# Splitting the columns of each batch 512 + 256 instead of 384 + 384 in a linear-attention, expert and feed-forward kernel

## The chip, the cores and the metric

One NeuronCore of a Trainium2 chip runs the program. The metric is device microseconds for one execution; the median of three runs is given beside the profiled execution. Engines are called PE (matrix products), DVE (vector), ACT (scalar), POOL (GpSimd) and SP (the queue that issues most transfers).

## The reference

```
# q, k, v: 2 batches, 8 heads, 768 places, 64 wide; blocks of 64 places
intra = (q_b @ k_b^T) * lam**(i - j)            # inside a block, i >= j
out_b = intra @ v_b + (q_b * lam**(i+1)) @ state
state = lam**64 * state + (k_b * lam**(63-i))^T @ v_b
x = out, heads side by side                     # 1536 tokens x 512
p = domain_probs / (sum + 1e-9)                 # 4 experts
x = sum_e p_e * (relu(x @ w1[e]) @ w2[e])       # 512 -> 1024 -> 512
h = x @ w_in;  out = (h * cos(h)) @ w_out       # 512 -> 2048 -> 512
```

All of it is in 32-bit floats. The kernel handles attention in 6 blocks of 128 places (`BLOCKS`), each for 2 batches (a unit is one block of one batch, 12 in all).

## The kernel before

Every number that goes into a product of the two later stages is split into a high part, rounded to the fast 32-bit matmul format, and a low part that is what is left. A product is then three matmuls: high by high, low by high, high by low. Copies to the high part are made by ACT, subtractions for the low part by DVE or POOL. All engines wait on semaphores by hand-written counts; the order on each engine is the order of the code.

**Attention.** DVE first makes two decay tables by running products along 128 places (`tensor_tensor_scan`): eight scans for `dmask`, from which `kpow` is copied, and four for `qpow`. Their input `lam` is loaded by ACT's queue while SP's queue loads q, k and v. Then, by block pairs p = 0 to 5, PE runs `scores`, `from_state`, `from_scores`, `decayed_state` and `increment`; DVE multiplies scores by the mask (`mask`, line 624) and makes parts of x and of the sums of x (`x_parts`, lines 645 to 653); ACT makes high parts (`x_high`, `t_high`); POOL multiplies q by `qpow` (`q_decay`, line 339) and makes low parts of the sums (`t_low`, line 345). The weights of the first quarter are split into high and low between these (`w1_piece`, lines 438 and 659).

**Experts.** The hidden width of the four experts is walked in 16 quarters of 256. The first product of a quarter is a seven-product form of a 2 by 2 block product (P1, P6, P5, P2, P7, P4, P3, in this order), on x and on sums of its blocks; the sums are why the columns (tokens) come in two batches. Before, the 768 columns of a batch were two sides of 384, and a step is one side of one quarter: 32 steps. A step holds 7 first products of 6 matmuls each (line 962) and, between them, the second products (`down`, line 981) of the step before, 8 of 6 matmuls each, 384 columns wide. Which of these follow which first product is written out in `FOLLOW` (and `FOLLOW_LAST` for the last step). Three PSUM banks hold the seven products, five are a ring for the second products. ACT copies P1 from its bank to memory (line 517), DVE adds it to P6 and P7 (lines 730 and 757), makes the four results (lines 715), applies relu and the expert's share (line 720), and adds second products to `y` (`down`, line 700). ACT makes the results' high parts (line 504), POOL their low parts (`h_low`, line 406). PE waits at the head of a product: P6 of side 1 for both pieces of the second weights (`w2_count(q, 1)`), P7 for DVE's sum with P6, P4 for DVE's sum with P7, and so on.

**Feed-forward.** 48 products of 4 x 3 matmuls of 512 columns (line 1040), each with two second products of 512 columns (line 1059). Their input is `y` of the experts, split again (`x2_high`, `x2_low`). The first of them waits for all low parts of the first side, of which DVE makes the second batch (line 706) and POOL the first. The eight second products of the last expert step stand among the first two of the 48.

```
FOLLOW = ((), (), (0,), (1, 2), (3, 4), (5, 6), (7,))
FOLLOW_LAST = ((), (0, 1), (2, 3), (4, 5), (6, 7), (), ())
```

## Time and profile before

| | |
|---|---|
| median of 3 runs | 826.63 us (826.59 to 828.08) |
| profiled execution | 826.41 us, its span 824.6 us |
| PE busy | 810.4 us (98% of the span), 4788 matmuls |
| DVE busy | 586.1 us (71%) |
| ACT / POOL busy | 291.5 us / 235.6 us |
| attention | 0 to 51.7 us |
| experts | 51.7 to 549.4 us |
| feed-forward | 551.4 us to the end |

A matmul is shown with an end that is modelled, and the next one starts before it, so that the time one costs is the distance between starts and not the duration shown. The list of stages above is read off the starts of lines 962 and 1040.

### The profile page before, as it was taken

Reading aid. Unit: us, or ns where it says so; the run is one execution under the profiler, and the core shown is the slowest. Engines: PE = TensorE matmul, PEld = TensorE weight load, DVE = VectorE, ACT = ScalarE, POOL = GpSimd, SP = SyncE. Lnnn points to the kernel's source line nnn. Section 1 sums busy time; section 2 is a strip of 40 time slices with the busy share of each in tenths; the row PEclk is TensorE's granted clock in tenths of the full one; section 3 lists DMA queues with packets and bytes.
Section 4 is the critical chain, followed back from the end, with each engine's and each line's share of the span. In section 5 each row is a group of like instructions: output and inputs, shape, how many; then the busy total and the mean of one; then the engine's idle time right before and its main releaser. Section 6 shows DMA issues by size and latency. Waiting matters only on the chain.

```text
span 824.6 us, 12232 instructions
## 1 busy us (share of the span) xinstructions
PE 810.4 (98%) x4788; PEld 757.7 (92%) x4788; DVE 586.1 (71%) x1028; ACT 291.5 (35%) x552; POOL 235.6 (29%) x232
## 2 busy tenths in 40 slices
PE   8988999999999999999999999999999999999998
PEld 7878999999999999999999999988888888888886
DVE  5987767667667667667667667676777777877776
ACT  3742322222222222221221222246545455454542
POOL 3854443443442442442442442243000000000000
PEclk9999999999999999999999999999999999999999
DMA  8941211111111021011011011100001101110004
GB/s 302 325 144 52 65 27 39 36 68 40 29 36 39 26 77 39 26 39 39 27 38 40 27 28 40 36 27 22 30 27 39 39 26 34 30 39 27 1 0 153
DMA packets 19869, 44.88 MB, mean 54 GB/s; under 512 B 2344, under 2 KB 2392, under 8 KB 19812
## 3 DMA queue, kind: packets, MB, share of 16 engines
q1 hardware_dynamic: 19668, 44.10, 17.0%
q8 instruction: 38, 0.62, 0.3%
q14 instruction: 19, 0.16, 0.1%
q10 hardware_dynamic: 144, 0.01, 0.0%
HBM read 40.93 MB, written 3.17 MB: 53 GB/s over the span
## 4 chain that ended last, share of the span: by engine, by line
PE 93%; DVE 4%; issue 1%; DMA 1%; ACT 0%; DVEq 0%; SPq 0%
PE ps L981 32%; PE ps L962 28%; PE ps L1040 16%; PE ps L1059 16%; DVE att L624 1%; DMA att<-att_in 1%; PE ps L879 1%; DMA lam<-lam_in 1%; PE ps L929 0%; DVE att L609 0%; DVE x_lo L706 0%; DVE w_lo L664 0%; DVE temps L715 0%; DVE temps L720 0%; PE ps L916 0%
## 5 line engine op out<-in xcount | busy, mean ns | idle before, releaser
L406 POOL TENSOR_TENSOR h_lo<-temps,h_hi 128x384 fp32r<-128x384 f32 x128 | 137.4, 1074 | 298.7 <-ACT h_hi L504 295.9
L504 ACT ACTIVATE h_hi<-temps 128x384 fp32r<-128x384 f32 x128 | 67.3, 526 | 360.1 <-DVE temps L720 360.1
L700 DVE TENSOR_TENSOR y<-ps,y 128x384 f32<-128x384 f32 x240 | 132.4, 554 | 72.5 <-PE ps L981 71.8
L981 PE MATMUL ps<-h_hi,w_hi 128*128 128x384 f32 x512 | 171.2, 334 | 0.0
L981 PE MATMUL ps<-h_hi,w_lo 128*128 128x384 f32 x512 | 171.1, 334 | 0.0
L981 PE MATMUL ps<-h_lo,w_hi 128*128 128x384 f32 x512 | 171.1, 334 | 0.0
L962 PE MATMUL ps<-x_hi,w_hi 128*128 128x384 f32 x448 | 150.9, 337 | 4.3 <-DVE w_lo L664 2.5
L962 PE MATMUL ps<-x_lo,w_hi 128*128 128x384 f32 x448 | 150.3, 335 | 0.0
L962 PE MATMUL ps<-x_hi,w_lo 128*128 128x384 f32 x448 | 150.3, 335 | 0.0
L981 PEld LDWEIGHTS ps<-h_lo,w_hi 128*128 128x128 f32 x512 | 96.1, 188 | 0.1
L981 PEld LDWEIGHTS ps<-h_hi,w_hi 128*128 128x128 f32 x512 | 96.1, 188 | 0.1
L981 PEld LDWEIGHTS ps<-h_hi,w_lo 128*128 128x128 f32 x512 | 96.1, 188 | 0.0
L962 PEld LDWEIGHTS ps<-x_hi,w_hi 128*128 128x128 f32 x448 | 84.6, 189 | 5.8 <-issue 3.0
L962 PEld LDWEIGHTS ps<-x_lo,w_hi 128*128 128x128 f32 x448 | 84.5, 189 | 0.0
L962 PEld LDWEIGHTS ps<-x_hi,w_lo 128*128 128x128 f32 x448 | 84.5, 189 | 0.0
L839 DVE SCALAR_TENSOR_TENSOR temps<-temps,ps 128x512 f32<-128x512 int32 x48 | 33.0, 687 | 61.5 <-ACT temps L582 61.5
L1040 PE MATMUL ps<-x_hi,w_hi 128*128 128x512 f32 x192 | 74.8, 389 | 1.7 <-DVE x_lo L706 1.7
L1059 PE MATMUL ps<-h_hi,w_hi 128*128 128x512 f32 x192 | 74.8, 390 | 0.0
L1040 PE MATMUL ps<-x_hi,w_lo 128*128 128x512 f32 x192 | 74.8, 390 | 0.0
L1040 PE MATMUL ps<-x_lo,w_hi 128*128 128x512 f32 x192 | 74.8, 389 | 0.0
L1059 PE MATMUL ps<-h_lo,w_hi 128*128 128x512 f32 x192 | 74.8, 389 | 0.0
L1059 PE MATMUL ps<-h_hi,w_lo 128*128 128x512 f32 x192 | 74.7, 389 | 0.0
(83 smaller groups left out, 1120.6 us busy)
## 6 DMA issues: line engine op xcount, KB each, us to landing
w_raw<-w_in SPq DMA_DIRECT2D x96, 256.0 KB, 2.6
att<-att_in SPq DMA_DIRECT2D x24, 512.0 KB, 6.3
temps<-p_scr SPq DMA_DIRECT2D x4, 768.0 KB, 4.1
out<-y SPq DMA_DIRECT2D x12, 256.0 KB, 2.0
att<-dp_in SPq DMA_DIRECT2D x1, 24.0 KB
p_scr<-att SPq DMA_DIRECT2D x1, 24.0 KB
lam<-lam_in ACTq DMA_DIRECT2D x1, 6.0 KB, 4.7
```

The lines of the kernel that those rows point to most:

```text
L406: pool.tensor_tensor(hs_lo[:, s % 2, f, at], r_ring[:, n % R_RING, :], f32(hs_hi[:, s % 2, f, at]), ALU.subtract).then_inc(s_hlo, 1)
L504: act.activation(hs_hi[:, s % 2, f, CT * b:CT * (b + 1)], r_ring[:, n % R_RING, :], ACT.Copy).then_inc(s_hhi, 1)
L624: dve.tensor_tensor(masked[:, n % 2, par, :], ps[:, (2 * n + par) % S_BANKS, :], dmask[:, par, :, :].rearrange("p a n -> p (a n)"), ALU.mu ...
L700: dve.tensor_tensor(at, from_bank, at, ALU.add).then_inc(s_y, 1)
L839: dve.scalar_tensor_tensor(out=rr[:, t, :], in0=kf[:, t, :], scalar=-C1, in1=bank, op0=ALU.mult, op1=ALU.add).then_inc(s_r1, 1)
L879: mm = pe.matmul(ps[:, (2 * n + par) % S_BANKS, at], qk[own, s, 1, at], qk[own, s, 0, at], start=True, stop=True)
L962: mm = pe.matmul(ps[:, bank, 0:CT], ww[q % 2][:, of], xx[:, side, 2 * x + k, :], start=(opens and k == 0 and n == 0), stop=(k == 1 and n = ...
L981: mm = pe.matmul(ps[:, DOWN_BANK + g % DOWN_BANKS, 0:CT], ww[:, s // SIDES % 2, f, at], hh[:, s % 2, f, tokens], start=(f == 0 and n == 0) ...
L1040: mm = pe.matmul(ps[:, v % GATE_BANKS, :], ww[q % 2][:, of], xx[:, k, chunk(c)], start=(k == 0 and n == 0), stop=(k == KT - 1 and n == 2))
L1059: mm = pe.matmul(ps[:, GATE_BANKS + i % KT, :], ww[:, q % 2, f, at], hh[:, j % CHUNKS, f, :], start=(f == 0 and n == 0), stop=(f == 1 and ...
```

## The change

The sides become 512 and 256 columns of each batch: blocks 0 to 3 are side 0, blocks 4 and 5 side 1. A first product has 512 columns on side 0 and 256 on side 1. The second products of a step are taken over both batches together in pieces of 512 columns: 8 for side 0 (two pieces of columns by four of outputs), 4 for side 1. So a quarter has 84 first matmuls as before, half of 512 and half of 256 columns, and 72 second ones of 512 in place of 96 of 384. In the feed-forward nothing changes but where its input's high and low parts are made: each chunk of 512 columns is now awaited by itself.

Other edits: the load of `lam` is the first on SP's queue; the four `qpow` scans come after `mask(0)`, `mask(1)` and `k_decay(1)`; POOL runs `normalise` and two `q_decay` before `diag`; on DVE the last piece of the first weights, `w1_piece(0, 2)`, comes after `mask(11)`; on ACT `t_high(4)` comes after the copy of P1 of step 0; in step 0 the pieces of the second weights are split earlier; on side 1 PE waits for the second weights at P5, not P6; `FOLLOW_LAST` is gone.

```
-CT = SEQ // SIDES
+SIDE_BLOCKS = (4, 2)
+CTS = (512, 256)
+CT = 512
...
-FOLLOW = ((), (), (0,), (1, 2), (3, 4), (5, 6), (7,))
-FOLLOW_LAST = ((), (0, 1), (2, 3), (4, 5), (6, 7), (), ())
-DOWN = KT * BATCH
+FOLLOW = (((), (), (), (0,), (1,), (2,), (3,)), ((), (), (0,), (1,), (2, 3), (4, 5), (6, 7)))
+DOWNS = (8, 4)
...
+            sp.dma_start(lam[:, :], lam_in).then_inc(s_lam, 16)
             load_qk(0)
...
+            normalise()
+            pool.wait_ge(s_tab, PAIRS)
+            q_decay(2)
+            q_decay(3)
             pool.wait_ge(s_id, 1)
...
-            act.dma_start(lam[:, :], lam_in).then_inc(s_lam, 16)
...
-                if p:
+                if 0 < p < BLOCKS - 1:
                     t_high(p - 1)
-                if 0 < p < BLOCKS - 1:
                     new_state(p)
...
                 if s == 0:
+                    t_high(BLOCKS - 2)
                     t_high(BLOCKS - 1)
+                    w2_piece(0, 0)
                     h_high(s, 0)
-                    w2_piece(0, 0)
+                    w2_piece(0, 1)
                     h_high(s, 1)
...
+            for a in range(PAIRS):
+                dve.tensor_tensor_scan(qpow[:, a, :], lam[:, HEADS + a:HEADS + a + 1].to_broadcast([P, P]),
+                                       zeros, 1.0, ALU.mult, ALU.add).then_inc(s_tab, 1)
             mask(2)
...
-                if 2 <= p <= 4:
+                if 2 <= p <= 3:
                     w1_piece(0, p - 2)
                 if p + 1 < BLOCKS:
                     mask(2 * p + 3)
+                if p == 4:
+                    w1_piece(0, 2)
...
-                    mm = pe.matmul(ps[:, bank, 0:CT], ww[q % 2][:, of], xx[:, side, 2 * x + k, :],
+                    mm = pe.matmul(ps[:, bank, 0:CTS[side]], ww[q % 2][:, of], xx[side][:, 2 * x + k, :],
...
-                    pe.wait_ge(s_hlo, 4 * s + 3 + b)
+                    pe.wait_ge(s_hlo, 4 * s + (3 if side == 0 and b == 0 else 4))
...
-                    mm = pe.matmul(ps[:, DOWN_BANK + g % DOWN_BANKS, 0:CT], ww[:, s // SIDES % 2, f, at],
-                                   hh[:, s % 2, f, tokens], start=(f == 0 and n == 0), stop=(f == 1 and n == 2))
+                    mm = pe.matmul(ps[:, DOWN_BANK + g % DOWN_BANKS, :], ww[:, s // SIDES % 2, f, at],
+                                   hh[side][:, f, tokens], start=(f == 0 and n == 0), stop=(f == 1 and n == 2))
...
-                            pe.wait_ge(s_xlo, UNITS // SIDES * (side + 1))
-                            pe.wait_ge(s_tlo, BLOCKS // SIDES * (side + 1))
+                            pe.wait_ge(s_xlo, 2 * sum(SIDE_BLOCKS[:side + 1]))
+                            pe.wait_ge(s_tlo, sum(SIDE_BLOCKS[:side + 1]))
...
-                    if i == P6 and side == 1:
+                    if i == P5 and side == 1:
 
                         pe.wait_ge(s_wlo, w2_count(q, 1))
...
-                        pe.wait_ge(s_x2lo, KT * (c + 1))
+                        if c != 1:
+                            pe.wait_ge(s_x2lo, KT * (c // 2 + 1))
+                        else:
+                            pe.wait_ge(s_x2lo1, KT)
                     if v == 0:
-                        pe.wait_ge(s_x2lo1, KT)
                         pe.wait_ge(s_r, 4 * STEPS - 3)
```

Three places on DVE, in the order of its queue. The first is its start: before, the scans for `dmask` (L609), the copy to `kpow` (L612), the scans for `qpow` (L616), and then the masks (L624) and `k_decay` (L633). The scans are listed as SCALAR_TENSOR_TENSOR.

```order
L609 SCALAR_TENSOR_TENSOR att<-lam,att 128x128 x8
L612 COPY kpow<-att 128x8
L616 SCALAR_TENSOR_TENSOR att<-lam,att 128x128 x4
L624 TENSOR_TENSOR att<-ps,att 128x512 x4
L633 TENSOR_TENSOR att<-att,kpow 128x512
```

The same stretch of the changed kernel (its lines: L623 and L626 are the `dmask` scans and the copy, L633 the masks, L642 `k_decay`, L679 the `qpow` scans):

```order
L623 SCALAR_TENSOR_TENSOR att<-lam,att 128x128 x8
L626 COPY kpow<-att 128x8
L633 TENSOR_TENSOR att<-ps,att 128x512 x4
L642 TENSOR_TENSOR att<-att,kpow 128x512
L679 SCALAR_TENSOR_TENSOR att<-lam,att 128x128 x4
```

The `qpow` scans moved behind the first two masks and `k_decay(1)`. The second place is the end of the attention on DVE, before: `mask(10)`, the last piece of the first weights (L659), `mask(11)`, then `x_parts(4)`.

```order
L653 TENSOR_TENSOR x_lo<-ps,x_hi 128x2x128
L624 TENSOR_TENSOR att<-ps,att 128x512 x2
L659 TENSOR_TENSOR w_lo<-w_sum,w_hi 128x1024
L624 TENSOR_TENSOR att<-ps,att 128x512 x2
L645 TENSOR_TENSOR att<-att,ps 128x256
```

And changed, where L668 is that piece:

```order
L662 TENSOR_TENSOR x_lo<-ps,x_hi 128x2x128
L633 TENSOR_TENSOR att<-ps,att 128x512 x4
L668 TENSOR_TENSOR w_lo<-w_sum,w_hi 128x1024
L654 TENSOR_TENSOR att<-att,ps 128x256
L655 TENSOR_TENSOR att<-ps,att 128x256
```

The piece now stands behind both masks. The third place is step 0 and the start of step 1 on DVE. Before: the sum with P6 (L730), result 0 (L720), the sum with P7 (L757), result by result (L715, L720), and the two pieces of the second weights (L664) late among them.

```order
L730 TENSOR_TENSOR temps<-ps,temps 128x384
L720 SCALAR_TENSOR_TENSOR temps<-ps,temps 128x384
L757 TENSOR_TENSOR temps<-ps,temps 128x384
L715 TENSOR_TENSOR temps<-ps,temps 128x384
L720 SCALAR_TENSOR_TENSOR temps<-temps 128x384
L715 TENSOR_TENSOR temps<-ps,temps 128x384
L720 SCALAR_TENSOR_TENSOR temps<-temps 128x384
L664 TENSOR_TENSOR w_lo<-w_raw,w_hi 128x512
L715 TENSOR_TENSOR temps<-ps,temps 128x384
L720 SCALAR_TENSOR_TENSOR temps<-temps 128x384
L664 TENSOR_TENSOR w_lo<-w_raw,w_hi 128x512
```

Changed (L741 and L762 the sums with P6 and P7, L729 and L724 the results, L673 the pieces):

```order
L741 TENSOR_TENSOR temps<-ps,temps 128x512
L729 SCALAR_TENSOR_TENSOR temps<-ps,temps 128x512
L673 TENSOR_TENSOR w_lo<-w_raw,w_hi 128x512
L762 TENSOR_TENSOR temps<-ps,temps 128x512
L724 TENSOR_TENSOR temps<-ps,temps 128x512
L729 SCALAR_TENSOR_TENSOR temps<-temps 128x512
L673 TENSOR_TENSOR w_lo<-w_raw,w_hi 128x512
L724 TENSOR_TENSOR temps<-ps,temps 128x512
L729 SCALAR_TENSOR_TENSOR temps<-temps 128x512
L724 TENSOR_TENSOR temps<-ps,temps 128x512
L729 SCALAR_TENSOR_TENSOR temps<-temps 128x512
```

The first piece now stands ahead of the sum with P7, and the second behind the second result.

## Rows read from the trace of the kernel before

**Rows 1.** The page's chain that ended last, by engine.
```profile
PE 93%; DVE 4%; issue 1%; DMA 1%; ACT 0%; DVEq 0%; SPq 0%
```
**Rows 2.** Stretches: length, busy by engine (instructions), clock, DMA share, GB/s.
```profile
51.70:69.00 17.30, 12.96 (x62) 11.70 (x61) 11.68 (x23) 7.88 (x15) 12.37 (x10) 0.90 0.32 106
69.00:549.00 480.00, 480.00 (x2771) 480.00 (x2770) 327.76 (x603) 122.68 (x237) 180.01 (x182) 1.00 0.13 39
549.00:552.00 3.00, 1.32 (x7) 0.94 (x7) 3.00 (x5) 0.86 (x3) 1.15 (x1) 1.00 0.00 0
```
**Rows 3.** The page's groups: busy, mean ns of one, idle before.
```profile
L981 PE MATMUL ps<-h_hi,w_hi 128*128 128x384 f32 x512 | 171.2, 334 | 0.0
L839 DVE SCALAR_TENSOR_TENSOR temps<-temps,ps 128x512 f32<-128x512 int32 x48 | 33.0, 687 | 61.5 <-ACT temps L582 61.5
L1040 PE MATMUL ps<-x_hi,w_hi 128*128 128x512 f32 x192 | 74.8, 389 | 1.7 <-DVE x_lo L706 1.7
```
**Rows 4.** Stretches of PE alone: a part of the feed-forward.
```profile
600.00:800.00 200.00, 200.00 (x884) 1.00 0.10 27
```
**Rows 5.** Timeline, weight loads only: start, duration, instruction (merged where alike).
```profile
21.25 0.97 PEld L903 LDWEIGHTS ps<-att 128*128 128x128 f32 x8
...
51.71 0.19 PEld L962 LDWEIGHTS ps<-x_hi,w_hi 128*128 128x128 f32 x1 [0.17 <-issue]
51.82 0.19 PEld L962 LDWEIGHTS ps<-x_lo,w_hi 128*128 128x128 f32 x1
```
**Rows 6.** Timeline of all engines at the start of the attention.
```profile
5.41 2.63 DVE L609 TENSOR_TENSOR_SCAN att<-lam,att 128x128 f32<-128x128 f32 x8 [4.41 <-DMA lam<-lam_in]
...
8.16 1.36 DVE L616 TENSOR_TENSOR_SCAN att<-lam,att 128x128 f32<-128x128 f32 x4
...
9.44 1.26 DVE L624 TENSOR_TENSOR att<-ps,att 128x512 f32<-128x512 f32 x2
...
10.25 1.93 PE L879 MATMUL ps<-att 64*128 64x128 f32 x16 [2.81 <-DVE att L624]
...
12.10 1.93 PE L929 MATMUL ps<-att 128*64 128x128 f32 x16
...
12.78 2.95 POOL L339 TENSOR_TENSOR att<-att 128x512 f32<-128x512 f32 x2
...
13.96 1.16 PE L879 MATMUL ps<-att 64*128 64x128 f32 x16
```
**Rows 7.** A stretch of PE: length, busy (matmuls), granted clock, DMA.
```profile
10.45:13.86 3.41, 3.41 (x32) 0.50 1.04 378
```
**Rows 8.** The page's list of transfers: KB each, us to landing.
```profile
lam<-lam_in ACTq DMA_DIRECT2D x1, 6.0 KB, 4.7
```
**Rows 9.** Timeline of POOL, DVE and PE at the end of the attention.
```profile
46.00 2.36 POOL L345 TENSOR_TENSOR x_lo<-att,x_hi 128x1024 fp32r<-128x1024 f32 x1 [1.58 <-ACT x_hi L474]
46.28 3.15 DVE L659 TENSOR_TENSOR w_lo<-w_sum,w_hi 128x1024 fp32r<-128x1024 f32 x1
...
48.72 1.09 PE L929 MATMUL ps<-att 128*64 128x128 f32 x16
50.69 1.09 PE L929 MATMUL ps<-att 128*64 128x128 f32 x16 [0.88 <-DVE att L624]
...
54.72 0.42 DVE L645 TENSOR_TENSOR att<-att,ps 128x256 f32<-128x256 f32 x1 [1.82 <-ACT x_hi L469]
```
**Rows 10.** Timeline of PE in steps 0 and 1.
```profile
57.58 0.44 PE L962 MATMUL ps<-x_hi,w_hi 128*128 128x384 f32 x1 [1.14 <-DVE temps L730]
...
59.54 0.44 PE L962 MATMUL ps<-x_hi,w_hi 128*128 128x384 f32 x1 [0.65 <-DVE temps L757]
...
65.48 0.66 PE L962 MATMUL ps<-x_hi,w_hi 128*128 128x384 f32 x1 [2.54 <-DVE w_lo L664]
65.94 0.52 PE L962 MATMUL ps<-x_lo,w_hi 128*128 128x384 f32 x1
```
**Rows 11.** Timeline of DVE in the middle of the experts, a side-0 step.
```profile
313.55 1.22 DVE L659 TENSOR_TENSOR w_lo<-w_sum,w_hi 128x1024 fp32r<-128x1024 f32 x1
```

More of the change, by code:

```diff
@@ L613, in _ @@
                .then_inc(s_kpow, 1)
-            dve.wait_ge(s_zeros, 1)
-            for a in range(PAIRS):
-                dve.tensor_tensor_scan(qpow[:, a, :], lam[:, HEADS + a:HEADS + a + 1].to_broadcast([P, P]),
-                                       zeros, 1.0, ALU.mult, ALU.add).then_inc(s_tab, 1)
             def mask(n):
@@ L724, in _ @@
                 q, side = s // SIDES, s % SIDES
+                bank_a, bank_b, bank_c = (ps[:, i, 0:CTS[side]] for i in range(3))
+                p1, v2, v3 = (t[:, 0:CTS[side]] for t in (prod1, u2, u3))
                 if s % (4 * SIDES) == 0:
@@ L740, in _ @@
                     w2_piece(q + 1, 0)
-                if last:
-                    down(s - 1, 2)
-                    down(s - 1, 3)
-                else:
+                if side == 1:
                     down(s - 1, 0)
@@ L806, in _ @@
                     w2_piece(q + 1, 1)
+                    for d in range(KT):
+                        x2_low(d)
             def gate_low(v):
@@ L1016, in _ @@
                     product(s, i)
-                    for d in (FOLLOW if s < STEPS - 1 else FOLLOW_LAST)[i]:
+                    for d in FOLLOW[side][i]:
                         down(s - 1, d)
```

235 lines of the change are left out of this document (114 added, 121 removed).

## Prediction

> **What bounds the kernel now.** I read the chain that ended last first: 93% of it is PE [rows 1]. Then the stretches: from 69 to 549 us PE has no idle time at all, 2771 matmuls in 480.00 us [rows 2]. That makes 480.00 / 2771 = 173.2 ns from start to start for 384 columns; the 334 ns that the group shows for one [rows 3] has a modelled end and is not a price. In the feed-forward, 884 matmuls of 512 columns in 200.00 us [rows 4] are 226.2 ns (226.7 if the two at the edges of the stretch are left out; I use 226.6). So the rest can come only from two sources: the number and width of the matmuls, and the places where PE does stand. These are three: the attention (which ends at about 51.7 us), steps 0 and 1 (51.7 to 69 us: PE busy 12.96 of 17.30 us at a mean clock of 0.90), and the change to the feed-forward (1.32 of 3.00 us) [rows 2]. Waits of DVE, ACT and POOL in the middle cost nothing now.
>
> **Part 1, widths.** Before, the experts have 32 steps of 7 x 6 and 8 x 6 matmuls, 2880 of 384 columns: 2880 x 0.1732 = 498.8 us. After, 672 first and 1152 second ones have 512 columns, 1824 x 0.2266 = 413.3 us, and 672 have 256. The columns are the same in all; 384 instructions fewer is what is gained. From the two prices one column costs (226.6 - 173.2) / 128 = 0.417 ns, which leaves 173.2 - 384 x 0.417 = 13 ns for each matmul whatever its width. A matmul of 256 columns would then start 119.8 ns after its forerunner, 672 x 0.1198 = 80.5 us, and the sum is 493.8: 5.0 us less. No row has a 256-column matmul of this format. What bounds it from below is the slope; from above the nearest are weight loads of 128 columns, which each matmul needs: the first two of the experts start 0.11 us apart, and eight in the attention take 0.97 us from first start to last end, (0.97 - 0.19) / 7 = 0.111 us each [rows 5]. So a load fits under 120 ns, but closely. If the 13 ns come on top of a load of 112 ns, the price is 125 ns, 3.5 us more. The 188 to 190 ns that a load lasts in the rows is not its distance, since 384 columns come every 173 ns. I take 120, because loads and matmuls start together in the dense stretch.
>
> The Trainium skill, "TensorE: Matmul & The Clock Gate", section "Back-to-back issue gap", gives N / 2.4 + 2.5 ns for the distance, 162.5 ns at 384 columns. The rows show 173.2, so the trace doesn't agree for this format. By the page's fixed 2.5 ns, 384 instructions fewer would be worth 1.0 us and not 5.0. Its section "LDWEIGHTS (loading the stationary operand)" gives columns / 1.2, that is 107 ns for a load, against 107 ns of streaming at 256 columns.
>
> **Part 2, the start.** The scans of `dmask` begin at 5.41 us, when `lam` lands (4.7 us after its issue [rows 8]); then come the copy, the `qpow` scans (1.36 us) and only at 9.44 the first mask [rows 6]. PE waited 2.81 us for it, and after that its granted clock was 0.50 from 10.45 to 13.86 us [rows 7], the 1.2 GHz level: the two groups of 16 matmuls take 1.93 us, while the same scores take 1.16 us once the clock is back [rows 6]. With the `qpow` scans gone from there the mask can start at 9.44 - 1.36 = 8.1 us even if `lam` lands as late as now. If `lam` lands sooner, scores(0) are next, which end at 10.25 - 2.81 = 7.4 us, so no more than 1.8 us is to be had. The load of `lam` pushes all of SP's loads back by one issue, about 0.4 us; at worst scores(0) come by that much later. With a wait of about 1 us in place of 2.81 the clock probably holds, worth up to 2 x 0.8 = 1.6 us more. Against this stands the new place of the scans: 1.36 us before the second pair of masks, and `q_decay(2)` and `q_decay(3)` (2.95 us on POOL [rows 6]) can begin only behind them, at about 14 us, when before they began at 12.78; PE needs them at about 16. Of the 3.4 us at the first masks I keep 1.4 for the end of the attention: the middle of it also hangs on transfers, with the DMA share at 1.04 [rows 7]. Bounds 0 and 3.4. `diag` behind two `q_decay` and `normalise` ahead cost nothing: `decayed_state` needs `diag` at about 20 us, and POOL idles while it waits for the tables.
>
> **Part 3, the end of the attention.** `w1_piece(0, 2)` took 3.15 us on DVE at 46.28, where 1.22 us is its price in the dense part [rows 9, 11]: it ended only 1.1 us after POOL's `t_low` of 46.00, which had started first. So `mask(11)` came at 49.4 though scores(11) were done before the `from_scores` of 48.72 began, and the last `from_scores` waited 0.88 us [rows 9]. With the piece behind the mask the 0.88 us go, since `from_scores(10)` ends at 48.72 + 1.09 = 49.8. The piece is then done by about 50.4 and P6 needs it at 52. That side 0 now needs four blocks and not three costs nothing: the low parts of block 3 are those of the `t_low` of 46.00, which ends at 48.4 [rows 9]. Gain 0.9.
>
> **Part 4, steps 0 and 1.** PE stood 4.3 us in the 17.3 [rows 2]: 1.14 for the sum with P6, 0.65 for the sum with P7, 2.54 for the second weights' low part [rows 10], to which comes 0.16 us each that the modelled ends hide. After the longest, nine matmuls came every 320 ns (65.48, 65.94, then at 0.32 us) instead of 173: 1.3 us at the clock of 1.2 GHz [rows 2, 10]. With restarts of 0.1 that is 6.7 us in all. What is late next, in the old clock of times with PE starting at 50.8: `x_parts(5)` no longer waits for `t_high(4)` (1.82 us in [rows 9]) and ends at about 55.0; the sum with P6 is done at 55.7 and P7 is due at 56.4, no wait. The sum with P7 is due at 58.0, but `w2_piece(0, 0)` stands ahead of it at 57.3, while POOL's `t_low(5)` runs from about 56.5 to 58.9. As in part 3 the piece would end only after it, near 59.4. The sum (0.69 us, as other DVE instructions of 512 columns [rows 3]) lets P4 start at 60.2 instead of 57.8: 2.4 us. Without the block it would be 1.1. In step 1 the first second product waits for the low part of result 2, about 0.5 us. With restarts I get 2.9 us left of 6.7: gain 3.8, bounds 2 and 5.2.
>
> **Part 5, the change to the feed-forward.** PE stood 1.7 us for the last low part that DVE makes [rows 3], 1.8 with the modelled end. After, the first of the 48 products needs the low parts of chunk 0 alone, whose `y` is complete two thirds through step 31; chunk 1 is needed 10.9 us later, and DVE is done some 2.5 us after the step's end. Gain 1.8. What is late next is the wait for all of `y` ahead of product 3: by the old distances it has 0.3 us to spare. I price it at 0.
>
> **The dense part again.** A side-0 step is now 15.0 us, a side-1 step 15.9. The closest wait is on side 1 at P5, which needs the last result sum of side 0. P3 of side 0 ends 13.6 us into it; DVE is then busy with the piece of 1024 (1.22 us [rows 11]) until 14.9, the sum ends at 15.5, and P5 is due at 15.0 + 1.4 = 16.4. Margin 0.9 us. The sum with P7 on side 0 has 0.4 us: P7's end, 0.2, DVE 0.69, against a second product of 1.36. Neither waits.
>
> **Sum.** 5.0 + 1.4 + 0.9 + 3.8 + 1.8 = 12.9 us. The profiled execution had 826.41 us, 1.8 more than its span and 0.2 less than the median. 826.4 - 12.9 = 813.5 us.
>
> **Rivals.** (a) At 256 columns the load decides: 125 ns instead of 120, 3.5 us more, 817.0. For it: 0.111 us per load, no room for the fixed 13 ns behind it. Against it: the loads start with the matmul before them, so their ends are 8 ns early. (b) The start's gain dies in the middle of the attention. Transfers fill the queues and DVE is held by POOL again at other places; parts 2 and 3 bring 0.5 instead of 2.3, and in step 0 both effects of part 4 are at their worse bound (1.8 less): 817.1. (c) All goes well: the attention gains 2 us more and `w2_piece` is not held (1.4): 810.1. (d) Slower: a wait in every quarter. If POOL holds the piece of 1024 as it did at 46.28, 1.93 us more, the last sum of side 0 ends at 17.4 and PE stands 1.0 plus 0.1 for the restart at P5 in each of 15 quarters: 16.5 us, 830.0. It turns the result once it is over 12.9 / 15 = 0.86 us a quarter. Against it: in the dense part this piece took 1.22 us, since POOL starts there behind DVE; with the new order POOL's neighbours end 0.5 us ahead of it or begin after it. (e) A load can't be had faster than its 188 ns once the stream above it is shorter: 672 x 0.068 = 46 us, 859. The row of eight loads at 0.111 speaks against it.
>
> **How the numbers follow.** My forecast 0.55, (a) 0.14, (b) 0.15, (c) 0.09, (d) 0.04, (e) 0.03. A measurement of this kernel tells 0.2%, 1.65 us, from no change. Slower by more than that are (d) and (e), 0.06 with a little of (d) ending level; level 0.03; faster 0.91. The range takes in (c), (a) and (b) and their bounds: 809.5 to 819.5.
>
> **What would show it.** Part 1: the distance between two 256-column matmuls in a timeline of the dense part, 0.12 us or 0.125, or 0.19 for (e). Part 2: the first mask at 8 us, PE's clock at 1.00 from 10 to 14 us. Part 3: no wait between the last two `from_scores`, and the first expert matmul near 49.4 us. Part 4: PE's idle time behind the attention 2 to 3 us in all, most of it ahead of P4 of step 0, no stretch at a clock of 0.50. Part 5: no wait at the first matmul of the feed-forward. The prediction is wrong if PE's busy time in the dense part has holes again, or if the attention doesn't end sooner.

## The result and the profile after

The changed kernel takes **815.58 us** (median of 4 runs, 815.41 to 816.09), the one before 826.61 on the same chip (median of 4). The ratio is 0.9863, with an interval of 0.9846 to 0.988. The forecast was 813.5 with a range of 809.5 to 819.5. The profiled execution of after also had 815.58 us and a span of 813.8, against 826.41 and 824.6. Two executions of the kernels below, one of the start alone and one of the kernel before beside it, took about 1350 us at a mean granted clock of 0.56; they are left out of every figure.

The page of the kernel after first: the chain by engine, two groups of expert matmuls and one of the feed-forward (busy, mean ns of one, idle before), and the transfer of `lam`.

```profile
PE 96%; DMA 2%; DVE 1%; POOL 0%; issue 0%; ACT 0%; SPq 0%; DVEq 0%
...
L963 PE MATMUL ps<-x_hi,w_hi 128*128 128x512 f32 (+1 forms) x448 | 150.4, 336 | 2.5 <-DVE temps L762 2.2
L982 PE MATMUL ps<-h_hi,w_hi 128*128 128x512 f32 x384 | 150.5, 392 | 0.8 <-POOL h_lo L422 0.8
...
L1043 PE MATMUL ps<-x_lo,w_hi 128*128 128x512 f32 x192 | 74.7, 389 | 0.0
...
lam<-lam_in SPq DMA_DIRECT2D x1, 6.0 KB, 1.8
```

PE's share of the chain went from 93 to 96% [rows 1]. The wait of 1.7 us for DVE's low part at the first feed-forward matmul [rows 3] is gone, and `lam` is 1.8 us under way instead of 4.7 [rows 8]. Then the same stretches as in [rows 2]: steps 0 and 1, the dense part, the change to the feed-forward.

```profile
48.88:66.00 17.12, 13.85 (x68) 11.18 (x67) 14.86 (x24) 8.42 (x15) 10.85 (x7) 1.00 0.35 107
66.00:543.00 477.00, 477.00 (x2407) 406.94 (x2406) 328.22 (x543) 123.24 (x234) 177.44 (x187) 1.00 0.13 39
543.00:558.00 15.00, 14.99 (x67) 12.09 (x66) 11.05 (x18) 10.52 (x18) 4.82 (x5) 1.00 0.07 20
```

From 66 to 543 us PE never stands, so that rival (d), a wait in every quarter, is out. Behind the attention 3.27 us of idle time are left of 4.3 (by the modelled ends), and the clock is 1.00 in all three stretches.

**Where the 10.8 us of the span went.** I took every distance between the starts of two neighbouring expert or feed-forward matmuls in both traces and subtracted what that width costs in the dense part: 226.7 ns for 512 columns, 173.3 for 384, 120.0 for 256. What is left over sits in few places, and these give the table.

| term | forecast | measured |
|---|---|---|
| Part 1, widths: 384 matmuls fewer, 5.1, less 1.5 where the width changes | 5.0 | 3.6 |
| Parts 2 and 3: first expert matmul at 48.88 instead of 51.72 | 2.3 | 2.8 |
| Part 4, steps 0 and 1: waits, restarts (the 0.1 us or so that the matmul behind a wait takes more) and low clock, 6.9 before, 4.2 after | 3.8 | 2.7 |
| Part 5, change to the feed-forward: 1.9 before, 0.3 after | 1.8 | 1.6 |
| sum | 12.9 | 10.7 |

**The new cost is where the width changes.** PE in a side-1 step of the dense part (start, duration with the modelled end, instruction): the end of a product of 256 columns and the second product behind it.

```profile
314.47 0.28 PE L963 MATMUL ps<-x_lo,w_hi 128*128 128x256 f32 x1
314.59 0.28 PE L963 MATMUL ps<-x_hi,w_lo 128*128 128x256 f32 x1
314.71 0.40 PE L982 MATMUL ps<-h_hi,w_hi 128*128 128x512 f32 x1
314.95 0.40 PE L982 MATMUL ps<-h_lo,w_hi 128*128 128x512 f32 x1
315.18 0.39 PE L982 MATMUL ps<-h_hi,w_lo 128*128 128x512 f32 x1
```

Two matmuls of 256 columns start 0.12 us apart, as forecast. But the six of 512 columns that follow a run of narrow ones come after 233, 236, 228, 233, 230 and 227 ns in place of 226.7: 27 ns more. The first narrow one behind wide ones comes after 113 ns instead of 120. A pair of switches costs 20 ns, a quarter has 5 pairs, there are 16 quarters: 1.6 us (summed over all distances 1.5). Between two kinds of products of the same 512 columns, in the side-0 steps, the distance stays at 226 or 227 ns, so it is the width and not the change of line or operands.

**The start and the end of the attention.** All engines of after in order of time, as [rows 6] and [rows 9] show them of before.

```profile
2.65 2.63 DVE L623 TENSOR_TENSOR_SCAN att<-lam,att 128x128 f32<-128x128 f32 x8 [1.66 <-DMA lam<-lam_in]
...
7.17 1.29 DVE L633 TENSOR_TENSOR att<-ps,att 128x512 f32<-128x512 f32 x2 [1.67 <-PE ps L880]
...
8.00 1.16 PE L880 MATMUL ps<-att 64*128 64x128 f32 x16 [0.89 <-DVE att L633]
...
11.33 1.16 PE L880 MATMUL ps<-att 64*128 64x128 f32 x16 [1.14 <-DMA att<-att_in]
...
44.09 2.36 POOL L361 TENSOR_TENSOR x_lo<-att,x_hi 128x1024 fp32r<-128x1024 f32 x1 [1.93 <-ACT x_hi L489]
...
46.98 1.97 PE L930 MATMUL ps<-att 128*64 128x128 f32 x32
47.27 1.21 DVE L668 TENSOR_TENSOR w_lo<-w_sum,w_hi 128x1024 fp32r<-128x1024 f32 x1
```

And the stretch of [rows 7] again, PE alone (length, busy, granted clock, DMA share, GB/s):

```profile
10.45:13.86 3.41, 2.53 (x58) 1.00 1.03 414
```

The first mask waits for PE's scores at 7.17 us and not for the scans, and the 2.81 us of PE have become 0.89. PE's clock stays at 1.00 where it was 0.50. Next late are the loads (1.14 us at 11.33, and 1.09 at 23.00 for a mask whose `k_decay` waited 1.04 us for a load). At the end the last 32 matmuls of `from_scores` run in one piece, and `w1_piece(0, 2)` behind the mask costs DVE 1.21 us instead of 3.15.

**Steps 0 and 1.** The waits of PE that are left, with what DVE and POOL did at the time.

```profile
52.20 4.74 POOL L361 TENSOR_TENSOR x_lo<-att,x_hi 128x1024 fp32r<-128x1024 f32 x2 [5.75 <-ACT x_hi L489]
...
55.26 2.23 DVE L673 TENSOR_TENSOR w_lo<-w_raw,w_hi 128x512 fp32r<-128x512 f32 x1
...
58.15 0.50 PE L963 MATMUL ps<-x_hi,w_hi 128*128 128x512 f32 x1 [2.18 <-DVE temps L762]
...
59.47 0.69 DVE L673 TENSOR_TENSOR w_lo<-w_raw,w_hi 128x512 fp32r<-128x512 f32 x1
...
62.88 0.36 PE L963 MATMUL ps<-x_hi,w_hi 128*128 128x256 f32 x1 [0.28 <-DVE temps L724]
...
64.65 0.50 PE L982 MATMUL ps<-h_hi,w_hi 128*128 128x512 f32 x1 [0.81 <-POOL h_lo L422]
```

The piece `w2_piece(0, 0)` takes 2.23 us while POOL works on its `t_low` of the last block, and ends 0.55 us behind it, at 57.49; its like at 59.47 takes 0.69. P4 waits for the sum behind the piece: 2.18 us and the restart.

### The profile page after: what moved, and what is told of

The parts are those of the page before. It is cut to its first block, busy times and chain, and to the rows that moved or that the text cites. A ratio compares the mean times of both kernels' runs of the same rounds, so it can differ in the third digit from the quotient of the medians.

```text
span 813.8 us, 11375 instructions
## 1 busy us (share of the span) xinstructions
PE 802.8 (99%) x4404; PEld 677.9 (83%) x4404; DVE 584.4 (72%) x964; ACT 292.0 (36%) x548; POOL 225.7 (28%) x228
## 4 chain that ended last, share of the span: by engine, by line
PE 96%; DMA 2%; DVE 1%; POOL 0%; issue 0%; ACT 0%; SPq 0%; DVEq 0%
PE ps L982 32%; PE ps L963 28%; PE ps L1043 16%; PE ps L1062 16%; DMA att<-att_in 2%; PE ps L880 1%; PE ps L930 1%; PE ps L904 1%; PE ps L917 1%; PE ps L894 1%; DVE w_lo L673 0%; DVE temps L729 0%; POOL h_lo L422 0%; DVE att L633 0%; DVE temps L724 0%
## 5 line engine op out<-in xcount | busy, mean ns | idle before, releaser
L422 POOL TENSOR_TENSOR h_lo<-temps,h_hi 128x512 fp32r<-128x512 f32 (+1 forms) x128 | 135.1, 1056 | 298.7 <-ACT h_hi L518 298.7
L518 ACT ACTIVATE h_hi<-temps 128x512 fp32r<-128x512 f32 (+1 forms) x128 | 67.3, 525 | 338.9 <-DVE temps L729 338.9
L712 DVE TENSOR_TENSOR y<-ps,y 128x512 f32<-128x512 f32 x180 | 124.1, 689 | 71.7 <-PE ps L982 71.7
L963 PE MATMUL ps<-x_hi,w_hi 128*128 128x512 f32 (+1 forms) x448 | 150.4, 336 | 2.5 <-DVE temps L762 2.2
L982 PE MATMUL ps<-h_hi,w_hi 128*128 128x512 f32 x384 | 150.5, 392 | 0.8 <-POOL h_lo L422 0.8
L963 PE MATMUL ps<-x_hi,w_lo 128*128 128x512 f32 (+1 forms) x448 | 150.5, 336 | 0.0
L963 PE MATMUL ps<-x_lo,w_hi 128*128 128x512 f32 (+1 forms) x448 | 150.5, 336 | 0.0
L982 PE MATMUL ps<-h_lo,w_hi 128*128 128x512 f32 x384 | 150.4, 392 | 0.0
L982 PE MATMUL ps<-h_hi,w_lo 128*128 128x512 f32 x384 | 149.4, 389 | 0.0
L982 PEld LDWEIGHTS ps<-h_hi,w_lo 128*128 128x128 f32 x384 | 72.1, 188 | 15.6
L1062 PE MATMUL ps<-h_hi,w_hi 128*128 128x512 f32 x192 | 74.8, 389 | 0.0
L1062 PE MATMUL ps<-h_lo,w_hi 128*128 128x512 f32 x192 | 74.7, 389 | 0.0
L1062 PE MATMUL ps<-h_hi,w_lo 128*128 128x512 f32 x192 | 74.7, 389 | 0.0
```

The lines of the kernel that those rows point to most:

```text
L422: pool.tensor_tensor(hs_lo[side][:, f, at], ring(s, i), f32(hs_hi[side][:, f, at]), ALU.subtract).then_inc(s_hlo, 1)
L518: act.activation(hs_hi[s % SIDES][:, f, at], ring(s, i), ACT.Copy).then_inc(s_hhi, 1)
L712: dve.tensor_tensor(at, from_bank, at, ALU.add).then_inc(s_y, 1)
L963: mm = pe.matmul(ps[:, bank, 0:CTS[side]], ww[q % 2][:, of], xx[side][:, 2 * x + k, :], start=(opens and k == 0 and n == 0), stop=(k == 1 ...
L982: mm = pe.matmul(ps[:, DOWN_BANK + g % DOWN_BANKS, :], ww[:, s // SIDES % 2, f, at], hh[side][:, f, tokens], start=(f == 0 and n == 0), st ...
L1062: mm = pe.matmul(ps[:, GATE_BANKS + i % KT, :], ww[:, q % 2, f, at], hh[:, j % CHUNKS, f, :], start=(f == 0 and n == 0), stop=(f == 1 and ...
```

## The experiments

The theory after the result: the four terms of the table are the four parts of the change, each works for its own reason, and the forecast was too high by the cost of the switches and by two waits in step 1. The rivals to it: that the terms are not separate, and that the widths carry more or less than the distances say. Five kernels put parts of the change into the kernel before or take the widths alone, six vary the changed kernel. The kernels come in three groups, each with its own executions of the kernel before, whose medians are 826.65, 826.67 and 827.37 us (the last for the widths alone, one wait for both chunks, and both improvements together). So a figure against before is the firmer one, and a figure against the change can be off by some tenths of a microsecond. The same holds for the end of the attention: the changed kernel and the five kernels that share its code up to there have the first expert matmul between 48.55 and 49.15 us.

**The start alone**, in the kernel before.

```diff
+            sp.dma_start(lam[:, :], lam_in).then_inc(s_lam, 16)     # ahead of all loads of SP
-            act.dma_start(lam[:, :], lam_in).then_inc(s_lam, 16)
 POOL: normalise, s_tab, q_decay(2), q_decay(3), then diag
 DVE:  qpow scans behind k_decay(1)
```

> The kernel before with the edits of the start alone: lam first on SP's queue, qpow scans behind mask(0), mask(1) and k_decay(1), POOL's normalise and two q_decay ahead of diag. In the changed kernel the first mask came at 7.17 us instead of 9.44, PE's clock did not fall, scores(4) came 2.5 us sooner, and the first expert matmul 2.8 us sooner. Theory (the start carries two thirds of that): 1.4 to 2.0 us less than the kernel before, first expert matmul at about 50.0 us. Rival (the start's gain is lost to transfers and to DVE held by POOL, and the end of the attention carries it): under 0.7 us less, though the first mask is sooner.

Measured: 823.16 us (median of five), ratio 0.9963 (0.995 to 0.9975), 3.1 us less by the ratio and 3.5 by the medians and the spans, more than either theory or rival said. The first expert matmul is at 49.50 instead of 51.72, 2.2 us sooner, where the prediction had 1.4. The rest comes from step 1. The last wait there in PE's timeline:

```profile
63.29 0.41 PE L962 MATMUL ps<-x_hi,w_hi 128*128 128x384 f32 x1 [2.54 <-DVE w_lo L661]
```

PE from 64 to 69 us (length, busy, clock, DMA share, GB/s) in this kernel, and under it in the kernel before:

```profile
64.00:69.00 5.00, 5.00 (x31) 1.00 0.29 67
```

```profile
64.00:69.00 5.00, 3.52 (x12) 0.66 0.32 105
```

The wait has the length that it had before, 2.54 us [rows 10], but this time the clock stays at 1.00 behind it: 1.3 us less. That differs between executions and not between the two kernels. Of the five of this kernel, three have a mean granted clock of 0.999 or 1.000 and take 822.8 to 823.2 us, two have 0.997 or 0.998 and take 824.2 and 824.6. Of the twenty of before, three have 0.997 or 0.998 and take 824.9 to 825.4; the others have 0.993 to 0.996 and take 826.4 or more. The kernel before has one stretch at the low clock at its start besides [rows 7]. Set like against like in this way (0.999 and 1.000 against 0.997 and 0.998; 0.997 and 0.998 against 0.996), the start alone is worth 2.1 to 2.2 us, which is what the first expert matmul shows.

**The end alone**, in the kernel before.

```diff
-                if 2 <= p <= 4:
+                if 2 <= p <= 3:
                     w1_piece(0, p - 2)
                 if p + 1 < BLOCKS:
                     mask(2 * p + 3)
+                if p == 4:
+                    w1_piece(0, 2)
 ACT: t_high(4) behind the copy of P1 of step 0
```

> The kernel before with the edits at the end of the attention alone: the last piece of the first weights behind mask(11) on DVE, t_high(4) behind the copy of P1 on ACT. Theory: the wait of 0.88 us between the last two from_scores goes, and x_parts(5) ends 2 us sooner, so that the wait for the sum with P6 in step 0 (1.3 us) goes too: 2.0 to 2.2 us less. Rival (the low part of the second weights, made late in step 0, is then waited for longer by what is won): 0.9 us or less.

Measured: 824.18 us, ratio 0.9975 (0.9963 to 0.9987), 2.5 us less by the medians and 1.9 by the spans, as the theory said and not the rival. The `from_scores` wait of 0.88 us is gone (first expert matmul at 50.64), and the sum with P6 makes PE wait 0.2 instead of 1.1 us, since `x_parts(5)` no longer waits for `t_high(4)`. The wait for the second weights grew to 2.7.

**The second weights' pieces alone**, in the kernel before.

```diff
 DVE, step 0:
                 weighted(s, 0, bank_a)
+                if s == 0: w2_piece(0, 0)
 ...
                 weighted(s, 1, ring(s, 1))
+                if s == 0: w2_piece(0, 1)
-  (both two results later)
-                    if i == P6 and side == 1:
+                    if i == P5 and side == 1:
```

> The kernel before with the edits of steps 0 and 1 alone: the second weights' pieces earlier on ACT and DVE, PE's wait for them at P5. Theory: the idle time of 2.7 us ahead of step 1's second product and the 1.3 us at the clock of 1.2 GHz behind it go, but the first piece is now held on DVE by POOL's t_low(5) ahead of the sum with P7, which costs 1.0 to 1.5 us: 2.5 to 3.0 us less in all. Rival (nothing is held): 4.0 us less.

Measured: 826.15 us, ratio 0.9996 (0.9986 to 1.0005): no change, and the theory missed. DVE and POOL in step 0 of this kernel:

```profile
57.94 2.37 POOL L345 TENSOR_TENSOR x_lo<-att,x_hi 128x1024 fp32r<-128x1024 f32 x1 [1.77 <-ACT x_hi L474]
...
58.42 2.44 DVE L664 TENSOR_TENSOR w_lo<-w_raw,w_hi 128x512 fp32r<-128x512 f32 x1 [0.39 <-ACT w_hi L448]
...
60.78 0.55 DVE L759 TENSOR_TENSOR temps<-ps,temps 128x384 f32<-128x384 f32 x1
```

The wait of 2.5 us in step 1 is gone, and one of 2.4 us ahead of P4 in step 0 took its place, with a stretch at the low clock behind it. Moved forward, the piece runs into POOL's `t_low`.

**All three together**, in the kernel before: the change without its widths.

```diff
 the edits of the three kernels above, SIDES of 384 and 384 as before
```

> The kernel before, sides of 384 and 384, with the edits of the start, of the end of the attention and of steps 0 and 1. What is left to the changed kernel are the widths and the chunk-wise wait of the feed-forward. Theory: 5.5 us less than the kernel before (attention 2.8, steps 0 and 1 2.7), about 821.1 us, and so 5.5 us more than the changed kernel: 1.6 from the feed-forward's wait, 3.6 from the widths. Rival (the order edits carry nearly all, the widths nothing since switches between 256 and 512 columns eat them): 8 to 9 us less than before.

Measured: 822.76 us, ratio 0.9956 (0.9941 to 0.9971), 3.9 us less. The first expert matmul is at 49.21, but `w2_piece(0, 0)` is held even longer than in the changed kernel:

```profile
52.08 4.72 POOL L345 TENSOR_TENSOR x_lo<-att,x_hi 128x1024 fp32r<-128x1024 f32 x2 [5.12 <-ACT x_hi L475]
...
54.64 2.70 DVE L661 TENSOR_TENSOR w_lo<-w_raw,w_hi 128x512 fp32r<-128x512 f32 x1 [0.39 <-ACT w_hi L449]
...
57.86 0.44 PE L964 MATMUL ps<-x_hi,w_hi 128*128 128x384 f32 x1 [2.70 <-DVE temps L761]
```

The start of POOL's work is fixed by the attention; a shorter product only brings P4, and the piece, closer to it. The low clock follows from 58.5 to 61.9 us, 1.5 us. Neither theory nor rival had this.

**The widths alone**: the changed kernel with start, end and pieces as before.

```diff
-            sp.dma_start(lam[:, :], lam_in).then_inc(s_lam, 16)
 POOL, DVE and ACT at the start, w1_piece(0, 2), t_high(4), w2_piece(0, 0) and w2_piece(0, 1): order of before
-                    if i == P5 and side == 1:
+                    if i == P6 and side == 1:
```

> The changed kernel with its start, its end of attention and its second weights' pieces as before: what is left of the change are the sides of 512 and 256 columns, the second products of 512 and the feed-forward's wait for one chunk alone. Theory: the widths are worth 5.15 us less the switch between widths (20 ns a pair, 80 pairs, 1.5 us), 3.6 net, and the feed-forward's wait 1.6: 5.2 us less than before, 821.4. Rival, the sum as predicted: 5.0 + 1.8 = 6.8 less, 819.8. Other rival: the run with the three other edits at sides of 384 was 3.9 us faster than before, and the whole change 11.0; if the parts add up, the widths alone must be worth 7.1 (819.5), and 2 us of that would sit in steps 0 and 1, where longer steps give DVE and POOL more room ahead of each wait: PE's idle time from the last from_scores to 69 us would then be 3 us or less instead of 4.3.

Measured: 822.35 us (820.03 to 823.53), ratio 0.9937 (0.9924 to 0.9949), 5.0 us less, next to the 5.2 of the theory. But its profiled execution, one of the two slowest (823.52 us, by the spans 2.9 less than the profiled one of before), shows that this is a balance. PE's longest wait in the list of waits, and its first one in the timeline:

```profile
PE ps L962 <- DVE w_lo L677: 3.6, 1, 3.6
```

```profile
10.44 2.08 PE L879 MATMUL ps<-att 64*128 64x128 f32 x16 [3.52 <-DVE att L637]
```

Widths and feed-forward bring 3.6 and 1.6 us. The first expert matmul comes 1.2 us later than before (52.95), since in this execution the clock at the start is 0.50 for 6.8 us, from 9.36 to 16.18, and not for 3.4. The excess of steps 0 and 1 (what their distances are above the price of their widths) is 8.0 us, 1.1 more: the late pieces now cost 3.6 us and not 2.5, with the low clock behind (0.50 up to 74.2 us, some 2.5 us). The rival, that the longer steps shorten these waits by themselves, is false: PE's idle time from 52.9 to 69 us is 4.6 us. The parts don't add up: the early pieces are worth nothing at 384 and 384, but with the widths changed this kernel's excess in steps 0 and 1 is 3.8 us over that of the full change: the wait for these pieces and the low clock behind it are some 6 us together, where the full change has 3.8 us of waits ahead of P4 and in step 1. How much of the 3.8 is the low clock's luck isn't separated; the one execution of this kernel with a mean clock of 0.998 took 820.03 us.

**The pieces one result later** than in the change.

```diff
                 weighted(s, 0, bank_a)
-                if s == 0: w2_piece(0, 0)
 ...
                 weighted(s, 1, ring(s, 1))
-                if s == 0: w2_piece(0, 1)
+                if s == 0: w2_piece(0, 0)
 ...
                 weighted(s, 2, ring(s, 2))
+                if s == 0: w2_piece(0, 1)
```

> The changed kernel, but on DVE in step 0 the two pieces of the second weights stand behind the results 1 and 2 and not ahead of the sum with P7. In the changed kernel PE waits 2.3 us ahead of P4 of step 0, while the first piece takes 2.23 us on DVE beside POOL's t_low(5), in place of 0.69. Theory (the piece is held by POOL, and the sum with P7 behind it): the wait falls to about 1.0 us (the sum's own time and the hand-over), and the change in step 1 (waits of 0.44 and 0.97 us) is small: 1.0 to 1.4 us less than the changed kernel. Rival (another wait takes its place, on the results that are made later or on the low parts in step 1): under 0.5 us less.

Measured: 814.15 us, ratio to before 0.9851 (0.9838 to 0.9864), 1.4 us less than the change. The wait ahead of P4 fell from 2.34 to 0.95 us, since POOL is done before the piece starts, and the piece takes 0.68 us. Side 1's P5 waits 1.58 instead of 0.44, and the 0.97 of the first second product is gone. The wait at P5 ends with the sum of result 3, which stands on DVE behind the second piece. PE's weight load and matmul at P5 of step 1:

```profile
58.68 0.68 DVE L673 TENSOR_TENSOR w_lo<-w_raw,w_hi 128x512 fp32r<-128x512 f32 x1
...
62.66 0.19 PEld L963 LDWEIGHTS ps<-x_hi,w_hi 128*128 128x128 f32 x1 [1.59 <-DVE w_lo L673]
62.70 0.36 PE L963 MATMUL ps<-x_hi,w_hi 128*128 128x256 f32 x1 [1.42 <-DVE temps L724]
```

**Fewer switches**: side 1's second products in 3 groups instead of 5.

```diff
-FOLLOW = (..., ((), (), (0,), (1,), (2, 3), (4, 5), (6, 7)))
+FOLLOW = (..., ((), (), (0, 1), (), (2, 3, 4), (), (5, 6, 7)))
 (DVE adds them to y in the same order)
```

> The changed kernel, but on side 1 the eight second products of 512 columns stand in three groups of 2, 3 and 3 (behind P5, P7 and P3) and not in five; DVE takes them in the same order. So in each quarter PE goes from 256 to 512 columns three times, not five. In the changed kernel the first matmuls of 512 behind a group of 256 come after 233, 236, 228, 233 and 230 ns instead of 227, and the first of 256 after 113 instead of 120: 0.02 us for each pair of switches. Theory (the switch costs, not the position): 2 x 16 x 0.02 = 0.64 us less. Rival (the longer groups make PE wait for DVE, or the cost is one of position): the same time or more.

Measured: 814.57 us, ratio to before 0.9855 (0.9841 to 0.9868), 1.0 us less. The distances say the same: 48 groups instead of 80, and their excess went from 1.5 to 0.9 us net. The price of a switch is thus shown by its number, 0.6 of the 1.0 us. The wait for `y` ahead of the fourth feed-forward product is gone too (0.3 us), and that makes up nearly all of the rest. In the profiled execution a low clock came back, after the same wait that the change had without it. PE of this kernel, a row of the timeline and then the stretch behind it:

```profile
58.29 0.50 PE L958 MATMUL ps<-x_hi,w_hi 128*128 128x512 f32 x1 [2.15 <-DVE temps L761]
```

```profile
59.57:62.90 3.33, 3.33 (x10) 0.50 0.33 98
```

It costs 1.6 us by the distances, and yet this execution is not slower for it. The waits of step 1, 0.44 us ahead of P5 and 0.97 ahead of the first second product in the changed kernel, are gone: PE comes there later and finds the work of DVE and POOL done. The excess of steps 0 and 1 is 4.2 us in both kernels. The four executions lie between 814.48 and 814.75 us at mean clocks of 0.998 to 1.000, and the one of the change at 0.998 took 815.41, no longer than the others.

**Half the weights' columns** in side 1's first products. This kernel leaves out rows 64 to 127 of each of them, so that its results are not those of the reference.

```diff
+                    rows = P if side == 0 else P // 2
-                    of = slice(FF2 * w + P * k, FF2 * w + P * (k + 1))
+                    of = slice(FF2 * w + P * k, FF2 * w + P * k + rows)
```

> The changed kernel, but the first products of side 1 (256 columns) use weights of 64 columns and not 128, so that half of their outputs are left out and the result is not the reference's. It asks what sets the 120 ns of such a matmul. Theory (a fixed 13 ns behind the streaming of 256 columns): still 120 ns. Rival (the weight load of 128 columns, 0.11 us, is what the next matmul waits for): 107 to 114 ns, and the first matmuls of 512 columns behind a group come after 227 ns, with no 233 to 236.

One execution: 812.29 us. The narrow products, and the wide one behind them:

```profile
314.79 0.28 PE L964 MATMUL ps<-x_hi,w_hi 128*64 128x256 f32 x1
314.91 0.28 PE L964 MATMUL ps<-x_lo,w_hi 128*64 128x256 f32 x1
315.02 0.28 PE L964 MATMUL ps<-x_hi,w_lo 128*64 128x256 f32 x1
315.13 0.40 PE L983 MATMUL ps<-h_hi,w_hi 128*128 128x512 f32 x1
315.37 0.40 PE L983 MATMUL ps<-h_lo,w_hi 128*128 128x512 f32 x1
```

The distance falls from 120 to 113 ns, so the theory (still 120) is false, and the number is the rival's. But its reason, that the load sets the distance at 256 columns, doesn't fit: with weights of 128 columns the distances at 256, 384 and 512 columns (120.0, 173.3, 226.7 ns) lie on one line, 0.417 ns a column and 13.3 ns on top. So the 13.3 ns is there at all three widths, and here, with weights of 64 columns, 113.3 - 256 x 0.417 leaves 6.7. What is on top goes with the columns of the weights; whether it does at other widths wasn't run. The six wide ones still come after 232, 236, 229, 232, 231 and 227 ns, so the rival's other half is false, and what they take more doesn't come from the narrow matmuls' loads. The first narrow one comes after 117 ns, 4 more than the others and no longer 7 less. What causes the cost of a switch stays open.

**`lam` on ACT's queue again**, the rest of the change as it is.

```diff
-            sp.dma_start(lam[:, :], lam_in).then_inc(s_lam, 16)
+            act.dma_start(lam[:, :], lam_in).then_inc(s_lam, 16)
```

> The changed kernel with the load of lam on ACT's queue as before. It should land at about 5.4 us and not at 2.6, so that the scans end at about 8.2 and the first mask comes at 8.2 to 8.3 instead of 7.2. Theory (from 12 to 23 us the stream of loads decides, one each 1.28 us, and scores(4) wait for theirs until 17.7 us): the first expert matmul moves by less than 0.4 us. Rival (the start is a chain through DVE and PE to the end of the attention): it comes 1.1 us later, and so does the end.

Measured: 816.74 us, ratio to before 0.9886 (0.987 to 0.9903), 1.2 us more than the change by the medians and 0.5 by the spans. `lam` lands 4.8 us after its issue. DVE and PE at the start, and then the stretch behind it with all engines (clock 0.50):

```profile
5.61 2.63 DVE L624 TENSOR_TENSOR_SCAN att<-lam,att 128x128 f32<-128x128 f32 x8 [4.61 <-DMA lam<-lam_in]
...
9.19 1.10 PE L881 MATMUL ps<-att 64*128 64x128 f32 x10 [2.15 <-DVE att L634]
```

```profile
9.60:13.00 3.40, 3.40 (x32) 2.85 (x30) 2.07 (x5) 0.90 (x4) 0.73 (x2) 0.50 1.01 396
```

PE waits 2.15 us and then runs 3.4 us at half its clock, and yet the first expert matmul comes only 0.6 us later (49.49), between the 0.4 of the theory and the 1.1 of the rival. The changed kernel waits for loads at 11.33 and 23.00 us and this one doesn't, so that the middle of the attention takes the rest back. Of the 2.2 us of the start the early transfer is thus the smaller part, 0.6 us; the order of the scans and of POOL, which this kernel keeps, is what is left, though no run has it alone.

**One wait for both chunks** at the feed-forward, as before.

```diff
                     if v == 0:
+                        pe.wait_ge(s_x2lo1, KT)
```

> The changed kernel, but the first matmul of the feed-forward waits for the low parts of chunk 1 too, as before it waited for both. Theory: the split of the wait by chunk is what removed it; DVE ends its low parts at 547.7 us and PE is there at 543.3, so PE stands some 4.4 us at this place and the kernel takes 4.0 to 4.5 us more, 819.6 to 820.1. Rival: only the 1.7 us that PE stood here before would come back, 817.3. Rival: nothing moves, because the wait for chunk 1 isn't what was removed.

Measured: 822.49 us, ratio to before 0.9936 (0.9922 to 0.995), 6.9 us more than the change. PE's wait there, and its stretch behind (clock 0.88 over all of it):

```profile
PE ps L1044 <- DVE x_lo L717: 4.6, 1, 4.6
```

```profile
540.00:550.00 10.00, 5.42 (x24) 4.29 (x23) 6.33 (x11) 3.44 (x7) 2.62 (x4) 0.88 0.11 29
```

The wait is as long as expected (4.7 us by the starts), far above the 1.7 of before: with the wider side 0 DVE has chunk 1 later. The expectation left out the low clock behind it, 13 matmuls of 405 to 427 ns, 2.6 us. Another low clock in step 0 (1.6 us) is no part of the loss: the waits of step 1 are gone for it, as in the run with 3 groups, and the excess of steps 0 and 1 is 4.2 us with it as without it. Against its own executions of before this kernel is 4.9 us faster where the change is 11.0, so that the loss is 6.1 us by that measure.

**Both improvements together**: the pieces one result later, and 3 groups.

```diff
 the edits of "the pieces one result later" and of "fewer switches"
```

> The changed kernel with both improvements found so far: the pieces of the second weights of step 0 one result later, and side 1's second products in 3 groups instead of 5. Apart they gave 1.4 and 1.0 us less than the changed kernel. Theory: they have nothing to do with each other, so 2.0 to 2.4 less, 813.2 to 813.6. Rival: part of the 1.0 came from waits in step 1, which both touch (the first second product is asked for in the same place); then 1.4 to 1.7 less, 813.9 to 814.2. Waits: 0.9 to 1.0 us ahead of P4 of step 0, 1.6 at P5 of step 1 as in the first of the two.

Measured: **813.36 us**, ratio to before 0.9829 (0.9817 to 0.9842), 2.2 us less than the change by the medians and 2.6 by the spans, of which 0.3 lie in the attention, whose code is the same. They add up, so the rival is false. The distances give 0.95 us ahead of P4 and 1.6 at P5 of step 1 over the price of the widths, as in the first of the two; the list of waits shows them by the modelled ends, and no third one behind the attention:

```profile
PE ps L958 <- DVE temps L724: 1.4, 1, 1.4
PE ps L958 <- DVE temps L759: 0.8, 1, 0.8
```

This is the fastest version.

## Why the prediction was right

The direction and the size within 2.1 us came out, and the range held. The widths are the largest term and the feed-forward the smallest, as forecast; the attention (2.8) and steps 0 and 1 (2.7), forecast at 2.3 and 3.8, are level. The sum is nearer than its terms by a little luck: 1.4 and 1.1 us too high in parts 1 and 4, 0.5 too low in parts 2 and 3. By its steps:

- **Part 1** was too high by 1.4 us, and it is the largest miss. Its number for a 256-column matmul, 120 ns, is what the trace shows. The step that failed is "the columns are the same in all; 384 instructions fewer is what is gained": it took the price of a matmul as independent of its neighbour's width. The table's 1.5 us at the switches are what it left out; the run with 48 groups instead of 80 shows them shrink with their number. The fixed 13 ns at any width is what the three widths show (13.3); that it falls to 6.7 with half the weights' columns is more than the working said. Rival (a) is out by its number, 120 and not 125. The 173.2 for 384 columns counts two matmuls at the edges of the stretch, which were left out for 512; it is 173.3, and the fewer instructions alone are worth 5.1 us and not 5.0.
- **Parts 2 and 3** were forecast at 2.3 and brought 2.8. Alone in the kernel before they moved the first expert matmul by 2.2 and 1.1 us; 1.4 for the start was mis-sized. In the changed kernel scores(4) start 2.6 us sooner (11.33 and not 13.96), and of the whole start 2.2 are left at the end of the attention in the run that has it alone: the step that gave up 2.0 of 3.4 us to the rest of the attention gave up too much. The bounds 0 to 3.4 held. The first mask came at 7.17, even before the 8 us of "what would show it". Rival (b), the gain dying in the middle of the attention, is out.
- **Part 4** had the mechanism and the place right: the wait ahead of P4, because `w2_piece(0, 0)` is held by POOL, was priced at 2.4 us and measured 2.3. What failed is the step "in step 1 the first second product waits for the low part of result 2, about 0.5 us": it was 0.97, and a wait of 0.44 ahead of P5 for a sum came on top that the working didn't name. With the restarts (0.4), which the working names but its 2.4 + 0.5 = 2.9 doesn't hold, 4.2 us are left. No stretch at the low clock came in this execution. That was not safe, as the run with 3 groups shows, but it would have cost nothing: the waits of step 1 take it up.
- **Part 5** was right: 1.8 forecast, 1.6 measured. The wait for all of `y` ahead of product 3, priced at 0 with a margin of 0.3 us, took 0.3 with its restart.
- **The dense part** had no wait, as worked out; the margin of 0.9 us at P5 and the 0.4 at P7 held. Rivals (d) and (e) are out: the distance of two narrow matmuls is 0.12 us although their loads last 0.19 in the rows.

The Trainium skill's page "TensorE: Matmul & The Clock Gate", section "Back-to-back issue gap", gives N / 2.4 + 2.5 ns for what it calls the isolated gap. The distances of this kernel are 226.7 ns at 512 columns and 120.0 at 256, where an estimate by the page would be 215.8 and 109.2; the measured ones decide. What no row told was that the two widths cost more side by side.

What the prediction hadn't asked, and the runs answered, is whether its parts could be taken apart. They can't in steps 0 and 1. The pieces alone brought nothing clear of the noise in the kernel before (0.5 us by the medians, ratio 0.9996), and the widths alone lengthened the wait for the second weights from 2.5 to 3.6 us. The sum of the parts came out because each wait was worked out in the changed kernel's own order, with what is late next, and not as an edit to the kernel before.

## What to carry to other kernels

Price a matmul by the distance of starts, and when widths are mixed count the switches as well: here 20 ns for each pair, which grouping like widths gives back. A step of DVE that is moved forward is worth what POOL does at its new time; look for POOL's long instruction there and put the step behind it. Work out the waits of a combined change in the order of the changed kernel, since edits that bring nothing alone can be what keeps another one's gain.

## What the runs showed of the hardware

- **Neighbours of another width.** Behind a run of 256-column matmuls six of 512 columns take 27 ns more in all (233, 236, 228, 233, 230, 227 against 226.7), and the first narrow one 7 ns less. With weights of 64 columns in the narrow ones the wide ones' 27 ns stay, and the first narrow one takes 4 ns more than the others.
- **What a matmul takes beyond its columns.** With weights of 128 columns 256, 384 and 512 columns take 120.0, 173.3 and 226.7 ns from start to start, 0.417 ns a column and 13.3 ns on top at each width. With weights of 64 columns and a width of 256 it is 113.3, 6.7 on top. At a granted clock of 0.50 they take 213 (the widths alone, from 69.3 us), 320 (before [rows 10]) and 427 ns (one wait for both chunks): 0.833 ns a column and nothing on top.
- **A wait of the same length isn't always followed by the low clock.** Behind 2.54 us in step 1 the kernel before fell to the 1.2 GHz level, and the run with the start alone did not. Behind 2.15 us ahead of P4 the run with 3 groups ran at 0.50 from 59.57 to 62.90, and the change, behind 2.18 us, kept 1.00. What tells them apart wasn't found, and executions of one kernel differ in it (the start alone: mean clocks of 0.997 to 1.000). Where nothing is late behind it, it costs 1.3 to 1.6 us (the start alone against before, all three together); where the next waits are for other engines, it can cost nothing (3 groups and one wait for both chunks, in step 0). The executions of the widths alone lie 3.5 us apart.
- **DVE beside POOL.** An instruction that makes the low part of 512 columns takes 0.68 us alone and 2.23 to 2.70 beside POOL's `t_low`, and it ends 0.54 to 0.55 us behind it in three kernels (this change, the pieces alone, the three edits together). The Trainium skill's page "SBUF — State Buffer", section "SBUF: two separate sides", describes a port pair that the two engines share and that one of them holds for a whole instruction; the rows agree with that.
- **A small transfer's place.** `lam`, 6 KB, takes 1.6 to 1.8 us as SP's first load and 4.7 to 4.8 on ACT's queue beside SP's loads.
